# Attention steps of the later batches in four slots instead of three, beside a mixer on one core

## The reference

```python
# attention: 8 heads of 48; a state of 48 x 48 for each head
state = alpha[:, :, t, :, None] * state + k[:, :, t] (outer) v[:, :, t]
y[:, :, t] = q[:, :, t] @ state
# mixer (x: 4 x 768 x 384)
h  = relu(x^T @ w_tok1) @ w_tok2 ;  u = x + h^T        # 768 -> 256 -> 768, over time
x2 = u + relu(u @ w_ch1) @ w_ch2                       # 384 -> 1536 -> 384
# channel mix, with x_prev = x2 one time step earlier
k = relu((mu_k x2 + (1 - mu_k) x_prev) @ w_k)          # 384 -> 1024
r = sigmoid((mu_r x2 + (1 - mu_r) x_prev) @ w_r)
out = r * ((k * k) @ w_v)
```

## Time and profile before

| | |
|---|---|
| median of 3 runs | 819.54 us (819.31 to 821.77) |
| the profiled execution | 819.78 us |
| its span, first to last instruction | 818.1 us |
| mean granted TensorE clock | 0.981 |
| VectorE, ScalarE, GpSimd busy | 504.3, 329.2, 189.6 us |
| first batch's attention alone | to about 58 us |
| mixers of batches 0, 1, 2 with attention | to about 482 us |
| last mixer, channel mix | to about 574, to 818 us |

### The profile page before, as it was taken

One profiled execution on the slowest core, in us unless ns is written; L12 is line 12 of the kernel. 1 busy time (PEld: TensorE's weight loads), 2 busy tenths in 40 slices (PEclk: granted clock), 3 DMA queues, 4 the chain that ended last, 5 costly groups with the idle time before them and its releaser, 6 DMA issues.

```text
span 818.1 us, 13704 instructions
## 1 busy us (share of the span) xinstructions
PE 755.0 (92%) x4598; PEld 735.7 (90%) x4598; DVE 504.3 (62%) x1307; ACT 329.2 (40%) x915; POOL 189.6 (23%) x318
## 2 busy tenths in 40 slices
PE   8975888898989898999889899999999999999998
PEld 7864888898989898988888899999899999999998
DVE  7963788875578888467887722133646645744751
ACT  4752433332244333244334313223535534633741
POOL 2780353333123423222332415100100000000000
PEclk9986999999999999999999999999999999999999
DMA  9834322242132332222324001401001101101000
GB/s 215 191 124 70 47 41 31 39 71 37 33 49 37 41 70 37 30 52 38 48 39 111 1 15 61 145 30 30 29 30 41 48 29 49 38 29 48 10 29 29
DMA packets 174026, 43.81 MB, mean 54 GB/s; under 512 B 161296, under 2 KB 171152, under 8 KB 173968
## 3 DMA queue, kind: packets, MB, share of 16 engines
q1 hardware_dynamic: 170720, 37.98, 23.2%
q0 software_dynamic: 1152, 4.72, 1.6%
q10 hardware_dynamic: 2096, 0.39, 0.3%
HBM read 33.63 MB, written 9.44 MB: 53 GB/s over the span
## 4 chain that ended last, share of the span: by engine, by line
PE 61%; DVE 23%; issue 7%; ACT 6%; SPq 1%; DMA 1%; POOL 0%; DVEq 0%; ACTq 0%
PE bank L761 12%; PE bank L687 12%; PE bank L671 11%; PE bank L739 11%; DVE qs_lo L1014 4%; ACT qs_hi L826 4%; PE bank L748 4%; DVE bank L974 3%; DVE decays L987 3%; DVE qkd L1004 3%; DVE decays L989 2%; PE bank L628 2%; PE bank L573 2%; PE bank L659 2%; DVE hid_lo L1069 2%
## 5 line engine op out<-in xcount | busy, mean ns | idle before, releaser
L1014 DVE SCALAR_TENSOR_TENSOR qs_lo<-qkd,rhead,qs_hi 96x128 fp32r<-96x128 f32 x144 | 88.6, 654 | 60.3 <-ACT qs_hi L826 60.3
L826 ACT ACTIVATE qs_hi<-qkd,rhead 96x128 fp32r<-96x128 f32 x144 | 50.0, 394 | 135.9 <-DVE qkd L1004 135.9
L1069 DVE SCALAR_TENSOR_TENSOR hid_lo<-bank,hid_hi 128x384 fp32r<-128x384 f32 x96 | 52.6, 548 | 77.6 <-ACT hid_hi L834 77.6
L834 ACT ACTIVATE hid_hi<-bank 128x384 fp32r<-128x384 f32 x96 | 45.7, 476 | 75.3 <-PE bank L671 75.3
L457 POOL TENSOR_TENSOR ks_lo<-qkd,ks_hi 96x128 fp32r<-96x128 f32 x72 | 34.6, 481 | 176.5 <-ACT ks_hi L830 176.5
L929 ACT ACTIVATE relu_k<-bank 128x384 f32<-128x384 f32 x64 | 31.5, 491 | 102.7 <-PE bank L739 85.1
L671 PE MATMUL bank<-u_lo,wch_hi 128*128 128x384 f32 x288 | 67.4, 342 | 0.0
L671 PE MATMUL bank<-u_hi,wch_hi 128*128 128x384 f32 x288 | 66.8, 340 | 0.0
L671 PE MATMUL bank<-u_hi,wch_lo 128*128 128x384 f32 x288 | 66.5, 339 | 0.0
L687 PE MATMUL bank<-hid_hi,wch_hi 128*128 128x384 f32 x288 | 66.4, 338 | 0.0
L687 PE MATMUL bank<-hid_hi,wch_lo 128*128 128x384 f32 x288 | 65.7, 335 | 0.0
(11 more groups left out here) (122 smaller groups left out, 1862.9 us busy)
## 6 DMA issues: line engine op xcount, KB each, us to landing
w_raw<-in_moe_w_ch SPq DMA_DIRECT2D x12, 384.0 KB, 3.2
x_scratch<-x_half POOLq DMA_DIRECT2D x8, 576.0 KB, 3.5
out<-x_half SPq DMA_DIRECT2D x24, 192.0 KB, 1.9
vt<-in_v SPq DMA_DIRECT2D x48, 72.0 KB, 2.2
qka<-in_q SPq DMA_DIRECT2D x49, 48.0 KB, 2.2
qka<-in_alpha SPq DMA_DIRECT2D x49, 48.0 KB, 2.2
qka<-x_scratch SPq DMA_DIRECT2D x4, 577.5 KB, 3.7
qka<-in_k SPq DMA_DIRECT2D x48, 48.0 KB, 2.2
```

The source lines that it names most:

```text
L826: nc.scalar.activation(dst[0:W2, h * P:(h + 1) * P], qkd[0:W2, first_of(i), :], ACT.Copy, scale=rhead[0:W2, i % 4, h:h + 1])\
L834: nc.scalar.activation(dst, b_ring[t % 2][:, 0:HT], func).then_inc(tile_hi, 1)
L1014: nc.vector.scalar_tensor_tensor(qs[1][0:W2, cols], qkd[0:W2, first_of(i), :], rhead[0:W2, i % 4, h:h + 1], qs[0][0:W2, cols], ALU.mult, A ...
L1069: ins = nc.vector.scalar_tensor_tensor(dst, src, 0.0, hi, ALU.max, ALU.subtract)
```

## The change

The steps of later batches are spread over four slots. `prepared_in(s)` names the step that is prepared in slot s: step 0 in slot 0, none in slot 1, step s-1 in slots 2 to 24. It is scored one slot later (for step 0 as for the others), applied two slots after its preparation and taken (`high_x`, `outputs`) three slots after it. TensorE's order within a slot is now mixer, scores, out (before: mixer, out, scores), with no scores ahead of slot 0's `token_up`. VectorE's is turn, outputs, scans and scale, first tile, split_low, second tile. ScalarE's is high_x, store_scores, first tile, spread_q with `ks_hi` ahead of the two `qs_hi`, second tile. GpSimd's is clear_future, own_head, add_x, prepare_x2, split_k, and a late piece in slots 4, 6 and 8 (before 4, 5, 6). `qs` and `ks` get two buffers, `split_low` waits for each half of `qs_hi` by itself. For the room, `w_raw` has three pieces instead of four, and three of `w_v`'s pieces are staged in `x_sum` instead of two. SyncE issues the first two halves of the second batch in slots 16, 19, 20 and 23 of the head.

```diff
-    NRAW = 4
+    NRAW = 3
+    NLATE = 3
-        qs = [sb(f"qs_{n}", [P, 2 * P], F32R) for n in ("hi", "lo")]
-        ks = [sb(f"ks_{n}", [P, P], F32R) for n in ("hi", "lo")]
+        qs = [sb(f"qs_{n}", [P, 2, 2 * P], F32R) for n in ("hi", "lo")]
+        ks = [sb(f"ks_{n}", [P, 2, P], F32R) for n in ("hi", "lo")]
...
+        def prepared_in(s):
+            if s == 0:
+                return 0
+            return s - 1 if 2 <= s <= STEPS else None
...
 # SyncE
-                for n in range(NRAW * c // 2, min(NRAW * (c + 1) // 2, NRAW)):
+                for n in range(2 * c, min(2 * c + 2, NRAW)):
                     load_piece(n)
...
+                if s % NP == 0 and s >= NP * (NC - 2) and s < STEPS:
+                    load_half(1, s // NP - NC + 2)
+                if s % NP == 3 and s >= NP * (NC - 2) and s < STEPS:
+                    load_half_v(1, s // NP - NC + 2)
                 for n in pieces_in(s):
                     if n + NRAW < NMIX:
                         load_piece(n + NRAW)
             for r in range(1, B):
-                for n in range(HALVES):
+                for n in range(2 if r == 1 else 0, HALVES):
                     load_half(r, n)
+                    load_half_v(r, n)
...
 # GpSimd
             def attention_part(r, s):
+                sc, yo = prepared_in(s - 2), prepared_in(s - 3)
+                if sc is not None:
+                    clear_future(r, sc)
                 if yo is not None and step(r, yo)[0] < NC - 1:
                     own_head(r, yo)
                 if yo is not None and step(r, yo)[1] == NP - 1:
                     add_x(r, step(r, yo)[0])
...
                     attention_part(r, s)
-                    if r == 1 and FIRST_UNIT <= s < FIRST_UNIT + NMIX - NEARLY:
-                        split_late(NEARLY + s - FIRST_UNIT)
                     if BASE_SLOT <= s < BASE_SLOT + 2 * KC:
                         prepare_x2(r - 1, s - BASE_SLOT)
+                    if prepared_in(s) is not None:
+                        split_k(r, prepared_in(s))
+                    late, odd = divmod(s - FIRST_UNIT, 2)
+                    if r == 1 and odd == 0 and 0 <= late < NMIX - NEARLY:
+                        split_late(NEARLY + late)
...
 # TensorE
             def attention_part(r, s):
+                sc, yo = prepared_in(s - 1), prepared_in(s - 2)
                 if sc is not None:
                     attention_scores(r, sc)
+                if yo is not None:
+                    attention_out(r, yo)
...
             for r in range(1, B):
-                attention_part(r, 0)
-                mixer_part(r - 1, 0)
-                for s in range(1, SLOTS):
+                for s in range(SLOTS):
                     mixer_part(r - 1, s)
                     attention_part(r, s)
...
 # ScalarE
+            def batch_slot(r, s):
+                tr, sc, yo = prepared_in(s), prepared_in(s - 2), prepared_in(s - 3)
+                if yo is not None:
                     high_x(r, yo)
+                if sc is not None:
                     store_scores(r, sc)
+                tile_first(r - 1, s)
                 if tr is not None:
                     spread_q(r, tr)
+                tile_second(r - 1, s)
...
                 if not is_first(r):
-                    act.wait_ge(scores_done, STEPS * r + i)
+                    act.wait_ge(scores_done, STEPS * r + i - 1)
+                    nc.scalar.activation(ks[0][0:W2, i % 2, :], qkd[0:W2, second_of(i), :], ACT.Copy)\
+                        .then_inc(ks_hi_ready, 1)
...
 # VectorE
-                dve.wait_ge(qbd_ready, 2 * (STEPS * r + i + 1))
                 for h in range(2):
                     cols = slice(h * P, (h + 1) * P)
+                    dve.wait_ge(qbd_ready, 2 * (STEPS * r + i) + h + 1)
...
+            def batch_slot(r, s):
+                tr, yo = prepared_in(s), prepared_in(s - 3)
+                if tr is not None:
+                    turn(r, tr)
+                if yo is not None:
+                    outputs(r, yo)
+                if tr is not None:
+                    scans(r, tr)
+                    scale_qk(r, tr)
+                tile_first(r - 1, s)
+                if tr is not None:
+                    split_low(r, tr)
+                tile_second(r - 1, s)
```

## The result

The changed kernel takes 757.46 us (median of 4 runs, 757.13 to 757.72), the kernel before 819.42 beside it: a ratio of 0.924 (95% interval 0.922 to 0.927). The gain is 62.1 us between the two profiled executions, 819.78 and 757.72. The forecast was 48.3; the time lies 14 us under it and 2.5 under the low end of the range.

A forecast was written before the change was run, and what follows sets the result against it. TensorE, busy 755.0 of 818.1 us, was taken as the bound, waiting for VectorE's qs_lo. Start -13.6, batch 1 -9.5 and batches 2 and 3 -25.2 sum to -48.3: from 819.78 to 771.5 us, range 760 to 790.

The forecast's parts named there:

- B: Steady slots: waits before the scores go and TensorE sets the slot; -14.5 us in each of batches 2 and 3.
- VectorE's line: VectorE's work for one steady slot, without any wait for y: about 4.05 us, against TensorE's slot of 4.47.
- D: Late weight pieces, batch 1 only: GpSimd holds qs_lo, the state comes late in slots 5, 7 and 9; 5.5 us lost.
- C: Slots 3 and 4 of every batch: new TensorE waits for a ring bank and the state; 1.9 us lost per batch.
- A: Start of the second batch's attention: early loads, token_up ahead of the scores, token_down at 62.8; 13.6 us gained.
- the late h1 tile: Start of batch 1: ScalarE takes the last two weight pieces 2 us later, which delays this tile; 0.5 us lost.
- The clock in batch 1: Batch 1: a second fall of TensorE's clock, taken at half its earlier cost of 3.6 us; 1.7 us lost.
- 1 (D nothing, no fall, 764): Batch 1: late weight pieces cost nothing and the clock doesn't fall; 764 us, chance 0.13.
- 2 (clock low until 75.5): Start: the clock stays low until about 75.5, as before, 6.8 us lost; 778 us, chance 0.12.
- 3: Start: loads don't come early, SyncE waits in its queue for a weight piece or a y; 785 us, chance 0.06.
- 4 (VectorE sets the slot): Steady slots: VectorE still sets them; at 4.95 us their whole gain is gone, 806 us, chance 0.07.
- 5 (both halves held in all slots, 844): Every slot: GpSimd holds both halves of qs_lo, VectorE needs 5.48 us; slower, 844 us, chance 0.03.

The follow-up runs named there:

- two thirds of the passes: Changed kernel with the third pass of channel_up and the second of channel_down left out, so that VectorE sets the slot: 677.93 us.
- the two gains together: Changed kernel with late weight pieces in slots 7, 10 and 13 and the second half's loads behind weight piece 12: 753.21 us.

## Why the prediction was wrong, point by point

The direction, the mechanism and the start were as forecast, the size was too small by 13.8 us. Two terms of the sum failed. B put the loss before the scores at 14.5 us a batch, and it was 16.0 and 16.3: the largest error, and the one that took the time out of the range. And VectorE's line was put at 4.05 us, and it is 3.48: this mis-sized D, and with it what C forecast. By the prediction's own steps:

1. **A, the start: right.** token_down at 62.87, forecast 62.8; clock low until 61.6, forecast some 4 us after 57.9. The second half's loads lasted until 55.9 (forecast 54.6), ScalarE took the last two pieces from 59.52 on (forecast 58.5), and the late h1 tile cost 0.97 and the refill, forecast 0.5.

2. **B, the steady slot: right in kind, the largest mis-sized term.** The forecast took the loss before the scores as 12.1 + 14 x 0.17 = 14.5 us a batch, with a slot of 4.47 without a gap as the measure. The loss can be summed directly. A step's scores follow the transposing matmul (the one with `qkd` and `ident`; the four steps of the last chunk have none). Two slots without a listed gap, before and after, timeline of TensorE:

```profile
249.57 0.25 PE L564 MATMUL bank<-ident,qkd 96*128 96x96 f32 x1
249.64 0.35 PE L573 MATMUL bank<-qs_hi,ks_hi 96*128 96x256 f32 x1
```
```profile
208.42 0.25 PE L585 MATMUL bank<-ident,qkd 96*128 96x96 f32 x1
208.45 0.36 PE L594 MATMUL bank<-qs_hi,ks_hi 96*128 96x256 f32 x1
```

   After, the two starts are 0.03 us apart in all 20 steps of batch 2; before they are 0.03 to 1.69 apart, and with the four steps of the last chunk the distances sum to 16.99 us. Less 20 x 0.03 and 4 x 0.09 (a y matmul stands ahead there), 16.0 us are lost, and in batch 3 16.3 (distances of 17.22). Of the 1.5 us more than forecast in batch 2, 1.0 lies in the ten steps whose waits are too short for the view of waits, and 0.5 in the fourteen listed: each lost 0.21 more than its figure, not 0.17. For the slot of 4.47 that served as the measure was itself waiting: its distance is 0.08, where 0.03 is no wait.

3. **C, new waits: mis-sized.** Forecast 1.9 a batch: a claim in slot 3, a claim and the state in slot 4. Measured are 0.59 in slot 1 and 0.50 in slot 4, 1.4 by the distance of starts, no wait for the state, and the old wait of slot 1 (0.49, 0.65 by the distance of starts), which was to remain, is gone. That is 1.1 less than forecast. VectorE's line is in this too: in slots 2 to 4 of batch 2 its periods from qs_lo to qs_lo were 3.96, 3.80 and 3.48 us, where 4.6, 4.6 and 4.05 were taken.

4. **D, the late pieces: failed, by VectorE's line.** The hold was as described, 2.97 us for both halves. Forecast was that the state comes 1.95, 1.5 and 1.5 late in three slots, 5.5 us; measured were 1.75 in slot 5, 0.55 in slot 7 and 0.10 in slot 9, 2.4 us. Slot 5 was not by the state alone. The timeline of VectorE and TensorE shows two waits:

```profile
78.89 2.62 DVE L1044 SCALAR_TENSOR_TENSOR qs_lo<-qkd,rhead,qs_hi 96x128 fp32r<-96x128 f32 x2 [0.63 <-ACT qs_hi L860]
```
```profile
81.61 0.35 PE L594 MATMUL bank<-qs_hi,ks_hi 96*128 96x256 f32 x1 [0.68 <-issue]
...
82.81 0.62 PE L616 MATMUL bank<-vt,relu_k 128*128 128x48 f32 x4 [0.61 <-POOL state L455]
```

   The held qs_lo ends at 81.51 and its scores follow at 81.61, 0.9 late: VectorE was so far behind there that even the longer lag didn't cover the hold. The state costs the other 0.85. What failed was the number under the forecast: VectorE's line of 4.05, which left it 0.3 to 0.35 a slot to make up a delay. The line is 3.48 (the run with two thirds of the passes shows it), and it makes up 0.9. Slots 6 and 7 show that this sets the price: VectorE's two periods are 3.48 and, with the hold, 5.84, together 9.32 us; TensorE needs 4.45 + 4.32 = 8.77; the difference is the 0.55 measured. With 4.05 for each it would have been 1.7.

   The 4.05 was put together from pieces of the earlier trace rows, and is 0.57 too long. Taken from start to start in the new order, the same parts are 0.36 (state and x_lo), 1.77 (transpose to the start of what follows qkd, against 2.04) and 1.35 (from there to the next transpose, against 1.45), with no handovers besides (against 0.15). Of the 0.27 in the middle, 0.18 is a handover that the new order fills: from the transpose's start to the next instruction's it is 0.68 in the earlier trace rows's slot, where a scan follows, and 0.50 after, where the state follows. The rest is in durations, which overlap the next start by some 0.08 each.

5. **The clock in batch 1: wrong in this execution.** 1.7 us were taken for a second fall; the windows of the kernel after (length, busy of five engines, clock, DMA share, GB/s) show none in the slots. In three of the variants that have the same stall it came (last section), so that it was absent here is in part luck:

```profile
58.00:62.00 4.00, 4.00 (x15) 4.00 (x15) 0.90 (x5) 2.17 (x5) 1.56 (x1) 0.55 0.88 289
62.00:66.00 4.00, 3.03 (x20) 2.62 (x19) 3.14 (x4) 1.43 (x5) 2.53 (x3) 1.00 0.48 143
74.00:178.00 104.00, 101.88 (x675) 100.65 (x675) 80.58 (x242) 45.37 (x156) 47.00 (x83) 1.00 0.36 52
```

The 13.8 us add up so, where more gain than forecast is plus: B 3 x 1.6 = 4.8 (batch 1 taken like the others), C 3 x 1.1 = 3.3, D 3.1, clock 1.7, the h1 tile -0.7; 12.2, and 1.6 over three batches are not assigned. Two of the terms, C's state wait and D, hang on VectorE's line; for C that is argued from the periods, and no run shows it apart.

The rivals: 1 (D nothing, no fall, 764) was nearest, with a D of 2.4 and the fall gone; 2 (clock low until 75.5) didn't come; 3 was made in the run with late loads and didn't occur by itself; 4 (VectorE sets the slot) has 0.9 us of room, not 0.4; 5 (both halves held in all slots, 844) fell: in the steady slots both halves take 0.35 us each (the group of qs_lo in the second batch has 341/346/350 ns min/median/max), and even with ks_lo ahead of x_half nothing was lost. The length of the hold was right, and its price was not, since the price is what the slack leaves of it. The rule that the forecast quoted from the Trainium skill, "SBUF — State Buffer", section "Who interferes with whom", says that the loser waits for the whole of the other's instruction. The trace agrees: qs_lo, 0.35 us alone, took 1.99 beside the subtraction of 1.84. That the first half was held through ks_lo and the cast behind it is more than the rule says.

The low end of the range, 760, was set from below by D and C at nothing (764, less 3.8) and took the 14.5 of B as known, though its 0.17 was read from one pair of slots. With the 1.6 us more in three batches it would have been about 755, and the measured time inside the range.

## What to carry to other kernels

When an operand is made an instant before it is used, move its use one slot later. Here that took away a loss of 16 us a batch, where freeing the maker from its holds alone left 7, and it made pairs held for 3 us free wherever the maker was ahead. Measure a loss by the distance of two starts over all repetitions, against a place that doesn't wait at all, not by the listed gaps. To know the slack of an engine, take its period from a stretch in which it never waits (or shorten the others' work until it sets the pace); a line added up from shown durations and the handovers of the old order came out 0.57 us too long, 16%. And before a difference of 2 to 5 us is given to an edit, see in the trace whether it lies behind the first instruction that the edit moves.

## What the runs showed of the hardware

- Between two GpSimd instructions a held VectorE instruction gets through, and the next is held again: the first half of qs_lo, begun 0.14 us before ks_lo's end, takes 1.05 until the gap behind the cast; the next takes 1.99 beside the subtraction of 1.84. Between ks_lo and the cast, where the profile shows no gap, it didn't get through. With nothing behind ks_lo, a half begun at the same place takes its usual 0.35 (the two gains together, at 92.73).
- TensorE's slow stretch at the start isn't fixed by the program: from 54 to 62 us the profiled executions show a granted clock of 0.60 and 0.55 (changed kernel), 0.72 and 0.85 (the two gains together) and 1.00 and 1.00 (second half's loads later, and tiles earlier), with the same instructions on TensorE; the last of these is, up to 57 us, the same program as the two gains together. In the stretch ahead of it, 50 to 54, TensorE was busy 3.08, 3.10, and 3.48 and 3.62 us in the same order: it had waited less where the clock didn't fall. In the channel mix some executions show a slow stretch of 3.4 us (changed kernel, 532.7 to 536.1, granted clock 0.50) and take 335.7 us from the last token_up on; those without it take 334.2. By half the clock a stretch of 6.8 us costs up to 3.4 (an estimate), so an effect of 2 to 3 us here is only as sure as its interval over several runs.
- Behind a stall of some 1.8 us in slot 5 the clock fell for 3.4 us in three variants (slot 6 has 6.01 us instead of 4.45 with the second half's loads later, 6.03 with late loads, 6.00 with single buffers), and didn't in two with the same stall, the changed kernel and the one with ks_lo first (4.45 both). So the stall alone doesn't decide whether the fall comes.
